# Splitting expert weights on GpSimd during the expert stage instead of ahead of it

## What is computed

```python
# 1: a gated recurrence over time, with a 40x40 state for each batch and head
C = f_stab * C + i_stab * outer(v_t, k_t);  n = f_stab * n + i_stab * k_t
y[t] = sigmoid(o_t) * (C @ q_t) / max(|n . q_t|, 1)
# 2: eight experts; each token goes to the one with the largest logit
logits = x @ w_gate;  expert_idx = argmax(logits, axis=1)
for e in range(8):                       # w1[e]: 320x1024, w2[e]: 1024x320
    h = maximum(x[mask_e] @ w1[e], 0.0)
    out[mask_e] = gate_w[mask_e] * (h @ w2[e])
# 3: a dense layer of width 2048
h = x @ w_in;  return maximum(0.01 * h, h) @ w_out
```

## Time and profile before

| | us |
|---|---|
| median of 3 runs | 961.06 |
| runs | 960.51 to 965.34 |
| the profiled execution | 962.15 |
| its span in the trace | 960.6 |
| TensorE busy | 777.8 (81%) |
| VectorE busy | 580.1 (60%) |
| ScalarE busy | 354.4 (37%) |
| GpSimd busy | 169.7 (18%) |

### The profile page before, as it was taken

One profiled execution on the slowest core, in us unless ns is written; L12 is line 12 of the kernel. 1 busy time (PEld: TensorE's weight loads), 2 busy tenths in 40 slices (PEclk: granted clock), 3 DMA queues, 4 the chain that ended last, 5 costly groups with the idle time before them and its releaser, 6 DMA issues.

```text
span 960.6 us, 18924 instructions
## 1 busy us (share of the span) xinstructions
PE 777.8 (81%) x6263; PEld 568.2 (59%) x6264; DVE 580.1 (60%) x1549; ACT 354.4 (37%) x643; POOL 169.7 (18%) x218
## 2 busy tenths in 40 slices
PE   0687766778696018999999998999999999999993
PEld 0566655656585017888888886555555555555552
DVE  7577777777676845666566665554545545455341
ACT  2366656556433302221222122334343343433431
POOL 4133233333333740000000000001000010100101
PEclk9788879887988559999999999999999999999997
DMA  3899999999740220333331300000000000000000
GB/s 108 229 236 298 318 314 321 309 312 280 226 120 21 104 84 24 137 130 130 130 122 49 116 15 2 1 1 28 1 8 21 1 27 0 25 3 0 29 1 27
DMA packets 51004, 103.41 MB, mean 108 GB/s; under 512 B 8174, under 2 KB 38574, under 8 KB 47886
## 3 DMA queue, kind: packets, MB, share of 16 engines
q1 hardware_dynamic: 47070, 89.74, 30.2%
q0 software_dynamic: 3888, 13.07, 4.1%
HBM read 74.93 MB, written 23.94 MB: 103 GB/s over the span
## 4 chain that ended last, share of the span: by engine, by line
PE 58%; DVE 15%; issue 10%; ACT 5%; DMA 5%; POOL 3%; SPq 2%; DVEq 1%; ACTq 0%; POOLq 0%
PE bank L1285 24%; PE bank L1376 13%; PE bank L1319 11%; DMA stage<-wB 4%; POOL d_x L522 3%; PE bank L1195 3%; PE bank L1170 2%; DVE slotB L839 2%; ACT X L702 2%; DVE qk L1108 1%; DVE sxt L1083 1%; PE bank L1275 1%; DVE dec L846 1%; DVE slotA L839 1%; PE bank L1179 1%
## 5 line engine op out<-in xcount | busy, mean ns | idle before, releaser
L1285 PE MATMUL bank<-X,slotA 128*128 128x512 f16 x768 | 181.3, 379 | 0.0
L1376 PE MATMUL bank<-slotB,dec 128*128 128x320 f16 x768 | 159.3, 299 | 16.1 <-DVE qk L1108 13.2
L1103 DVE TENSOR_TENSOR X<-bank,X 128x512 f32<-128x512 f32 x96 | 66.4, 692 | 105.5 <-ACT X L702 105.5
L1285 PE MATMUL bank<-qbd,slotA 128*128 128x128 f16 x1984 | 118.1, 221 | 3.4 <-DVE qbd L1036 3.4
L1285 PEld LDWEIGHTS bank<-qbd,slotA 128*128 128x128 f16 x1984 | 115.5, 99 | 6.3 <-issue 4.1
L1285 PEld LDWEIGHTS bank<-X,slotA 128*128 128x128 f16 x768 | 75.2, 98 | 74.1
L1376 PE MATMUL bank<-slotB,qk 128*128 128x320 f16 x384 | 114.8, 299 | 0.0
L1376 PEld LDWEIGHTS bank<-slotB,dec 128*128 128x128 f16 x768 | 73.0, 98 | 67.3 <-DVE qk L1108 23.8
L1319 PE MATMUL bank<-slotB,emov 128*128 128x320 f16 x496 | 102.1, 300 | 4.5 <-issue 2.3
L702 ACT ACTIVATE X<-bank 128x512 f32<-128x512 f32 x96 | 57.4, 598 | 129.3 <-PE bank L1285 129.3
L676 ACT ACTIVATE emov<-bank 128x512 f16<-128x512 f32 x62 | 37.0, 597 | 180.7 <-PE bank L1285 180.7
(11 more groups left out here) (196 smaller groups left out, 1293.5 us busy)
## 6 DMA issues: line engine op xcount, KB each, us to landing
stage<-wB SPq DMA_DIRECT2D x10, 1280.0 KB, 9.5
stage<-wA SPq DMA_DIRECT2D x10, 1024.0 KB, 5.7
d_wA<-slotA SPq DMA_DIRECT2D x6, 1280.0 KB, 11.3
d_wB<-slotB SPq DMA_DIRECT2D x6, 1280.0 KB, 14.2
slotA<-d_wA SPq DMA_DIRECT2D x6, 1280.0 KB, 5.6
slotB<-d_wB SPq DMA_DIRECT2D x6, 1280.0 KB, 5.5
stage<-wA SPq DMA_DIRECT2D x20, 256.0 KB, 6.5
num<-d_x POOLq DMA_DIRECT2D x31, 162.0 KB, 2.5
```

The lines of the kernel that those rows point to most:

```text
L1103: v.tensor_tensor(fgl[f % 2], bank[f % 2][:, :], ft[f % 2], ALU.max).then_inc(f_g, 1)
L1285: ins = t_.matmul(pf, a[:, col:col + P], x(k), start=(q == 0), stop=(q == len(ops) - 1))
L1376: ins = t_.matmul(bank[4 + q][:, 0:DM], x[f % 2][:, q * P:(q + 1) * P], slotB[2 + f // NF][:, c0:c0 + DM], start=(f == 0 and z == 0), stop ...
```

## The change

- Units 0 to 5 are no longer split during the recurrence, and neither stored nor loaded back; `d_wA` and `d_wB` are gone. Their squares, sums and scales stay there. `high` and `low` run there only for units 6 and 7, around chunk 3.
- A unit's load waits for the squares of the unit that had its half of `stage` (`next_unit`). The dense units are loaded in chunk 4 and squared two steps later than before.
- In the expert stage SyncE loads the float32 weights of experts 2 to 7 a second time, into the space of `X` (`eA`, `eB`), which is free once the tokens are scattered.
- GpSimd splits them (`split`): multiply by the scale in place, cast to the slot, subtract. It waits for `m_h` or `m_o` before it writes to a slot, and for its own instruction before each next one.
- ScalarE issues the token fetches, three pairs ahead, behind `x_high`.

```diff
-            def store_unit(u, s):
-                sp.wait_ge(lo_done, NSL * (u + 1))
-                sp.dma_start(d_wA[ds(u, 1)]..., slotA[s][:, :]).then_inc(split_stored[s], 16)
-                sp.dma_start(d_wB[ds(u, 1)]..., slotB[s][:, :]).then_inc(split_stored[s], 16)
...
+            def next_unit(c, b):
+                if b == 2 and not (isinstance(c, int) and c >= SPLIT_CHUNK):
+                    sp.wait_ge(sq_done, NSL * (2 * c + 1))
+                    load_unit(2 * c + 2, 0)
+                if b == 0 and not (isinstance(c, int) and not 1 <= c <= SPLIT_CHUNK):
+                    sp.wait_ge(sq_done, NSL * (2 * c))
+                    load_unit(2 * c + 1, 1)
+                if b % 2 == 0 and is_c(c, SPLIT_CHUNK + 1):
+                    sp.wait_ge(lo_done, NSL * (b // 2 + 1))
+                    load_unit(NE + b // 2, b // 2)
...
             for e in range(2, NE):
-                last = sp.value_load(tab_last[0:1, e - 2:e - 1], min_val=0, max_val=NPAIR)
-                sp.wait_ge(m_h, 2 * (last + 1))
-                sp.dma_start(slotA[e % 2][:, :], d_wA[e - 2]).then_inc(wA_landed[e % 2], 16)
-                sp.wait_ge(m_o, last + 1)
-                sp.dma_start(slotB[e % 2][:, :], d_wB[e - 2]).then_inc(wB_landed[e % 2], 16)
+                if e > 2:
+                    sp.wait_ge(exp_split, SPLIT_OPS * (e - 3) + SPLIT_A)
+                load_first(e - 2, eA, expA_landed)
+                if e > 2:
+                    sp.wait_ge(exp_split, SPLIT_OPS * (e - 2))
+                load_second(e - 2, eB, expB_landed)
...
+            def split(e):
+                ...
+                pool.wait_ge(expA_landed, 48 * (u + 1))
+                one_more(g.tensor_scalar(eA, eA, scA, None, ALU.mult))
+                pool.wait_ge(m_h, 2 * (last + 1))
+                ...
+                one_more(g.tensor_copy(a[:, 0:SA], eA))
+                ...
+                one_more(g.tensor_tensor(a[:, SA:SA + 2 * FE], eA[:, 0:2 * FE], a[:, 0:2 * FE], ALU.subtract))
+                ...
+                one_more(g.tensor_tensor(lo, eA[KR:P, 2 * FE:3 * FE], lo, ALU.subtract))
+                ...
+                g.memset(touch[:, 0:1], 0.0).then_inc(wA_landed[s], 16)
+                pool.wait_ge(expB_landed, 16 * (u + 1))
+                one_more(g.tensor_scalar(eB, eB, scB, None, ALU.mult))
+                pool.wait_ge(m_o, last + 1)
+                ...
+                one_more(g.tensor_copy(w[:, :, 0, :], x))
+                ...
+                one_more(g.tensor_tensor(w[:, :, 1, :], x, w[:, :, 0, :], ALU.subtract))
+                ...
+                g.memset(touch[:, 1:2], 0.0).then_inc(wB_landed[s], 16)
...
-                if b % 2 == 1 and c_prep(c) and at >= 3:
+                if b % 2 == 1 and is_c(c, SPLIT_CHUNK) and at >= 3:
                     if at == 3:
                         act.wait_ge(sc_chain, SC_UNIT * (2 * c + s + 1))
-                        if not is_c(c, 0):
-                            act.wait_ge(split_stored[s], 32 * c)
                     high(2 * c + s, s, s, at - 3)
...
+            def pair(p, i):
+                h_high(p, 1 - i)
+                x_high(p + 1, i)
+                if not (isinstance(p, int) and p + 3 >= NPAIR):
+                    fetch(p + 3, i)
```

More of the change, by code:

```diff
@@ L182, in build @@
         hi_done, lo_done = sem("hi_done"), sem("lo_done")
-        split_stored = [sem(f"split_stored{i}") for i in range(2)]
+        expA_landed, expB_landed, exp_split = sem("expA_landed"), sem("expB_landed"), sem("exp_split")
         rt = sem("rt")
@@ L379, in reload @@
                     load_o_late(*((c, b + 1) if b < B - 1 else (c + 1, 0)))
-                if unit is not None:
-                    sp.wait_ge(lo_done, NSL * (unit + 1))
-                    load_unit(unit + 2, b // 2)
+                next_unit(c, b)
                 store_x(st - 2, (b + 2) % NBUF)
@@ L525, in _ @@
             pool.wait_ge(x_done, NST)
-            def fetch(p, i):
-                t = pool.value_load(tab_tile[0:1, ds(p, 1)], min_val=0, max_val=NST - 1)
-                pool.dma_start(xt[i], d_x[ds(t * P, P), :]).then_inc(xt_landed[i], 16)
             pool.wait_ge(rt_tab, 1)
-            for p in range(2):
-                fetch(p, p)
-            pool.wait_ge(lo_done, NSL * NU)
+            pool.wait_ge(lo_done, NSL * 4)
+            g.memset(touch[:, 4:8], 0.0)
             for i in range(2):
-                for w in (wA_landed, wB_landed):
-                    g.memset(touch[:, :], 0.0).then_inc(w[i], 16)
-                    pool.wait_ge(w[i], 16)
+                g.memset(touch[:, i:i + 1], 0.0).then_inc(wA_landed[i], 16)
+                g.memset(touch[:, 2 + i:3 + i], 0.0).then_inc(wB_landed[i], 16)
+                pool.wait_ge(wA_landed[i], 16)
+                pool.wait_ge(wB_landed[i], 16)
             for i in range(2):
@@ L552, in _ @@
+            for e in range(2, NE):
+                split(e)
             pool.wait_ge(rt, RT_TOK)
@@ L607, in job @@
                 s = b // 2
[L608 removed]
+                u = unit_of(c, b)
+                if u is not None:
+                    h = b // 2 if c_prep(c) else 1 - b // 2
                     if b % 2 == 0 and at >= 2:
@@ L676, in h_high, with fetch @@
                     a.activation(hh[i][:, q * 512:(q + 1) * 512], bank[2 * i + q][:, :], ACT.Relu).then_inc(m_hh, 1)
+            def fetch(p, i):
+                t = act.value_load(tab_tile[0:1, ds(p, 1)], min_val=0, max_val=NST - 1)
+                if not (isinstance(p, int) and p < 2):
+                    act.wait_ge(xs_done, p - 1)
+                act.dma_start(xt[i], d_x[ds(t * P, P), :]).then_inc(xt_landed[i], 16)
+            act.wait_ge(scattered, 16 * NST)
+            act.wait_ge(rt_tab, 1)
+            act.wait_ge(x_done, NST)
+            fetch(0, 0)
+            fetch(1, 1)
+            fetch(2, 0)
             x_high(0, 0)
+            fetch(3, 1)
             h_high(0, 0)
             x_high(1, 1)
-            with act.Fori(1, NPAIR - 2, 2) as p:
+            def pair(p, i):
[3 more added lines that the diff above has]
+                    fetch(p + 3, i)
+            with act.Fori(1, NPAIR - 4, 2) as p:
                 for i in range(2):
-                    h_high(p + i, 1 - i)
-                    x_high(p + i + 1, i)
+                    pair(p + i, i)
+            for p in range(NPAIR - 4, NPAIR - 2):
+                pair(p, 1 - p % 2)
             h_high(NPAIR - 2, 1)
@@ L890, in lows @@
             def lows(c, b, g):
-                for on, u, s in ((b >= 2 and c_prep(c), 2 * c, 0), (b < 2 and c_after(c), 2 * c - 1, 1)):
+                for on, u, s in ((b >= 2 and is_c(c, SPLIT_CHUNK), 2 * c, 0), (b < 2 and is_c(c, SPLIT_CHUNK + 1), 2 * c - 1, 1)):
                     if on and (b % 2 == 0 or g < 2):
@@ L1247, in step @@
                     to_state(u, g, f, st)
-                if b % 2 == 1 and (c_prep(c) or is_c(c, PREP_CHUNKS)):
-                    sums(2 * c + b // 2, b // 2, st)
+                u = unit_of(c, b)
+                if b % 2 == 1 and u is not None:
+                    sums(u, b // 2 if c_prep(c) else 1 - b // 2, st)
             def chunk(c):
@@ L1437, in c_prep, with unit_of @@
     return not isinstance(c, int) or c < PREP_CHUNKS
-def c_after(c):
-    return not isinstance(c, int) or 1 <= c <= PREP_CHUNKS
+def unit_of(c, b):
+    if c_prep(c):
+        return 2 * c + b // 2
+    if (c == PREP_CHUNKS and b >= 2) or (c == PREP_CHUNKS + 1 and b < 2):
+        return NE + (1 - b // 2)
+    return None
 def buf(c, b):
@@ L1457, in for_chunks @@
     chunk(0)
-    with eng.Fori(1, PREP_CHUNKS) as c:
+    with eng.Fori(1, SPLIT_CHUNK) as c:
         chunk(c)
-    for c in range(PREP_CHUNKS, NC):
+    for c in range(SPLIT_CHUNK, NC):
         chunk(c)
```

91 lines of the change are left out of this document (51 added, 40 removed).

## The result

The changed kernel takes 1021.5 us (median of four, 1018.7 to 1023.8) beside 962.4 us of the kernel before: a ratio of 1.061, 95% interval 1.057 to 1.066. The forecast of 1002 us had the sign and was 19.5 us short.

| stretch | before | after | difference |
|---|---|---|---|
| start to the last step (last L880, L938) | 301.64 | 262.28 | -39.4 |
| that step to the end of the last scatter's issue | 44.8 | 43.9 | -0.9 |
| end of that issue to the first reduction of `x_scale` | 5.8 | 11.8 | +6.0 |
| that reduction to the last `y_add` | 245.2 | 338.1 | +92.9 |
| dense layer and output | 363.1 | 360.9 | -2.2 |

What follows compares the result with a forecast made beforehand. The recurrence was taken as bound by DMA, the expert stage by TensorE. 962.15 - 36 (recurrence) + 75 (VectorE held off) + 2 (first fetch) = 1003 us profiled, so forecast 1002 us; range 965 to 1050.

Steps and rivals of the forecast that it cites:

- Where the time goes: Expert stage: TensorE would wait for `x_scale`, not for weights, with VectorE "busy" up by some 90 us.
- Recurrence, -36 (25 to 50): Recurrence, steps 3 to 16: without the twelve stores, 124 us in place of 162.5, of which 36 are kept as gain.
- GpSimd's chain, 22 us (20 to 38): Expert stage: GpSimd's seven split instructions for one expert sum to 22 us, 3.2 us an instruction.
- rival B: Expert stage: GpSimd slower with one input, chain 28 us and 1031 us, or chain 38 us and 1077 us; chance 0.13.
- How long VectorE is held off, 15.4 us of 22: Expert stage: VectorE held off for 0.70 of each chain; each expert loses 12.4 us, six lose 75.
- half an instruction before the first and a whole one before each of the other four: `x_scale`: waits of 1.6 us once and 3.2 us four times a pair, 14.4 us of waiting in 20.6.
- rival D: Expert stage: half of the waits, as VectorE gets two instructions into each GpSimd gap; 48 us lost, 975 us; chance 0.12.
- What VectorE gives back, 3 us a chain: Expert stage: pairs outside the chain give back VectorE's idle time and its lead of one pair, some 3 us.
- First fetch, +2 (-1 to +4): Before the expert stage: fetch leaves 1 us earlier but shares the DMA engines with 2.8 MB of weights, +2 us.
- The fetch on ScalarE's queue, nothing: Expert stage: token fetches issued by ScalarE behind `x_high`, 7 us before use against 2.5 us to land, cost nothing.
- A: Expert stage: lock hardly bites, one-column instructions slip through GpSimd's gaps; +14 us instead of +75, 942 us; chance 0.15.
- C: Recurrence gains 10 us instead of 36, from short DMA rows or ScalarE's squares; steps near 150, 1028 us; chance 0.06.

Runs made afterwards that it cites:

- e3: Changed kernel with each of GpSimd's seven split instructions per expert cut to one column, waits and loads kept: 926.6 us, expert stage 244.7 us.
- e2: Changed kernel with `x_scale`'s three one-column instructions given one tensor input and its two wide multiplies moved to ScalarE: 931.8 us, expert stage 251.8 us.
- e6: Changed kernel with twelve stores of 1,280 KB put back into the recurrence, without the halves: 1047.5 us, steps 3 to 16 in 156.4 us.
- e7: Kernel before, halves kept, with stores and loads back cut to 32 columns: 958.4 us, steps 3 to 16 in 160.1 us.
- e9: Changed kernel with GpSimd's two multiplies given a second operation, times 1.0: 974.7 us, expert stage 295.4 us, chain 21.6 us.
- e5: Changed kernel with other forms of GpSimd's two multiplies for experts 3 to 6 (broadcast, constant, copy, two operations): 1004.9 us.
- e1: Changed kernel with the three one-column, two-input instructions of `x_scale` given one tensor input and pointer scalars: 958.3 us, expert stage 273.7 us.
- e4: Changed kernel with GpSimd's seven split instructions per expert replaced by memsets, which write and don't read: 970.2 us, expert stage 285.6 us.
- e8: Changed kernel with GpSimd's seven split instructions per expert cut into 30 pieces of 512 or 640 columns: 955.9 us, expert stage 273.4 us.
- e11: Changed kernel with the edits of e2, e9 and e10 together: 921.1 us beside 960.9 us of the kernel before, ratio 0.958.
- e10: Changed kernel with SyncE issuing the first expert weights only once the first two token fetches have landed: 1016.0 us.

## Why the prediction was right in sign and short in size

**Where the time goes.** Right. TensorE waits for `x_scale`, and VectorE's "busy" rises by 106 us where 90 were named. TensorE never waits for slots; e3 excludes DMA, e2 shows the port.

**Recurrence, -36 (25 to 50).** The sum was right, -39.4, from other places, and so in part by luck: steps 3 to 16 gave 28.7 us (133.8 and not 124 us remain), and 10.6 us came from the steps ahead of 3 (3.5) and behind 16 (7.1), where the prediction counted nothing. Ahead of step 3 the kernel before has 8 high and 5 low halves that are gone. Behind 16 the split work is nearly the same, but in before the steps wait more there. Of the two neighbours of the step of 9.7 us, only the one ahead of it takes "a little more", as the prediction read (10.9 us); the one behind it takes 13.0, and 7.6 in the changed kernel. The reason was half right: the prediction called the stretch bound by DMA and gave nearly the whole gain to the stores. By e6 and e7 the halves were a bound of about the same size, and stores alone would have given 2 us (4 by the last step). The step that failed is reading a DMA share of 1.00 as the only bound, without asking how fast the split itself would let a step be. It did no harm since the change removes both. In the changed kernel, from 220.68 to 242.00 us, TensorE is busy all the time at a DMA share of 1.00, which shows the same from the other side.

**GpSimd's chain, 22 us (20 to 38).** 31.1 us. The casts came as taken (0.89 ns a column; 0.85), the two-input forms too (2.0; 2.2). The two multiplies were mis-sized: 8.02 and 6.76 us, 2.6 ns a column and not 0.85. The trace of before has no such instruction, and both bounds were taken from rows of other operations: the lower from a memset, the upper from a `tensor_tensor`, rival B's 1.39 from an affine select. The true rate lay above even the 2.26 of the slow bound; only the casts kept the sum under 38 us. The Trainium skill, page "GPSIMD Engine Reference", section "Engine selection", calls one-input forms roughly line-rate. The casts and the two-operation multiply here agree (0.89 and 0.92 ns); the one-operation multiply doesn't.

**How long VectorE is held off, 15.4 us of 22.** Too much: 18.3 us of 31.1 (110 / 6), and 10.4 of 21.6 in e9. The step that failed is "half an instruction before the first and a whole one before each of the other four". In after there are 34 long waits in the 15 pairs that a chain meets, 2.3 a pair and not five: L1083 waits in 15 pairs, L1084 in 6, L1086 in 2, L1087 in 4, L1089 in 7. A pair loses 110 / 15 = 7.3 us, 1.65 mean instructions of GpSimd (4.44 us) and not 4.5; in e9, with 12 pairs, it is 1.7 of 3.08 us. The number of pairs was off the other way: the prediction lets a chain of 22 us meet 22 / 20.6 = 1.1 pairs, 6 in all. It took the chain to run in one piece, but GpSimd waits for its slot, for 10 to 30 us behind the first multiply in four of six chains and for 6 us behind the second in four, and so it meets 15 pairs, some of them with a single instruction. In the gap between two GpSimd instructions two one-column instructions slip through, as at 364.88 and 365.16. That was rival D's mechanism, two in a gap. Its formula (2 instructions a pair, the chain in one piece) with the measured chain gives (31.1 x 0.59 - 3) x 6 = 92 us (GpSimd's mean instruction 4.44 us, waits of 2 x 4.44 = 8.9 in 6.2 + 8.9), and with e9's chain 47 us; measured are 93 and 50. That it comes so close is partly luck, since both its waits for a pair (2 instructions) and its pairs (2 a chain) are off. The forecast's formula with the measured chain would have given 124 us.

**So two errors met.** By the forecast's formula the slow multiplies are worth +49 us (75 to 124), and the overpriced waiting -31 (124 to 93). Their sum is the 18 us by which the stage was short; a forecast within 2% of the time was partly luck.

**What VectorE gives back, 3 us a chain.** The size agrees, (110 - 93) / 6 = 2.8, but the books have one more entry, which the prediction left out: the clock. In TensorE's books the +92.9 us are +70.2 idle and +22.7 busy at a lower mean clock. The two sides are not to be added; they describe the same 93 us. By run:

| | VectorE's five lines, us more (pairs hit) | TensorE idle, more | TensorE busy, more | clock | stage, more |
|---|---|---|---|---|---|
| after | 110 (15) | 70.2 | 22.7 | 0.88 | 92.9 |
| e5 | 90 (13) | 59.2 | 20.0 | 0.88 | 79.1 |
| e9 | 62 (12) | 31.7 | 18.5 | 0.91 | 50.2 |
| e1 | 60 (24), the two wide lines | 21.7 | 6.8 | 0.95 | 28.5 |
| e4 | 39 (9), the two wide lines | 23.9 | 16.6 | 0.92 | 40.4 |
| e8 | 42 (22) | 19.8 | 8.4 | 0.94 | 28.2 |
| e11 | none on the port | -0.4 | 1.8 | 0.97 | 1.4 |

e1 and e9 hold VectorE off about equally long, and e9's stage loses 22 us more. In e9 the lost time falls on fewer pairs: L1083 waits long in 12 pairs, in e1 in 24. One reading is that each pair hit gives back VectorE's idle 1.28 us of the earlier trace rows (24 x 1.28 = 31, 12 x 1.28 = 15) and that shorter single gaps leave TensorE at its clock. The first half fits after (19, measured 17), e1 (31; 31) and e9 (15; 12), but not e4, which loses in the stage all that VectorE is held off (12; -1), nor e8 (28; 14). So this is argued and doesn't cover every run; what decides how much comes back stays open, and no run separated the idle time from the clock.

**First fetch, +2 (-1 to +4).** +6.0, above the bound. The mechanism was named, the size was not: the fetch was charged a share of the DMA engines' time and not a place behind more than half of the weights. e10 shows it.

**The fetch on ScalarE's queue, nothing.** Right in the loop: e3's stage is 244.7 us.

**Rivals.** A (one-column instructions slip through, 942) needs one-tensor forms; e1 makes them so and reaches 958 us, 16 more than A's price. B's slow GpSimd was true for the multiplies. C fell: steps 3 to 16 took 133.8 us and not near 150. D was right that two instructions pass in a gap; its time of 975 us is 46 us short, since it took the forecast's chain.
